# A gated two-network kernel: the hidden rows of the first network turned by VectorE and sixteen transfers a block instead of by TensorE

## The chip, the cores and the metric

One Trainium2 core runs the whole program in one launch. The metric is device microseconds (us) of an execution; the median of several runs stands for a kernel. Engines are named as in the profile: PE (TensorE matmul), PEld (its weight loads), DVE (VectorE), ACT (ScalarE), POOL (GpSimd) and SP (SyncE, which here only issues transfers).

## The reference

```python
for t in range(S):                                   # linear attention, 4 x 8 heads, S = 768, D = 48
    state = alpha[:, :, t, :, None] * state + einsum('bhd,bhe->bhde', k[:, :, t], v[:, :, t])
    y[:, :, t] = einsum('bhd,bhde->bhe', q[:, :, t], state)
...                                                  # x: 3072 tokens x 384
expert_idx = argmax(logits, axis=1)                  # one of 8 experts for each token
for e in range(8):                                   # first network
    h = maximum(x[mask] @ w1[e], 0.0)                # 384 -> 1024
    out[mask] = gate_w[mask, None] * (h @ w2[e])     # 1024 -> 384
h = out @ w_in                                       # second network, 384 -> 2048
return maximum(0.01 * h, h) @ w_out                  # 2048 -> 384
```

## The kernel before

The kernel has three stages: the attention (to about 120 us of the span), the first network (about 137 to 435 us) and the second network (to the end). The change lies in the first network.

Tokens are sorted by expert into 31 blocks (the code's windows) of 128 tokens. Every engine runs its own program over the 31 blocks, in a loop of two blocks a turn with a few blocks written out at either end, and semaphores order the engines. `w` is the block, `u` its parity, `half` one half (512) of the 1024 hidden features. For a block, in the order of the work:

- POOL gathers 128 rows of 384 (`gather`), PE turns them in three 128x128 pieces (`turn_gx`), ACT rounds them to the matmul's type (`gx_round`) and DVE takes the remainder (`gx_rest`), so that each product runs as three matmuls of parts.
- PE multiplies by w1 into two banks (`hidden`, 9 matmuls of 512 columns for each half), ACT writes the ReLU to `hs` (`relu`).
- PE turns `hs` in eight 128x128 pieces into two banks (`turn_h`), ACT rounds (line 780), DVE takes the remainder (line 1192); together these are `hT`.
- PE multiplies by w2 (`contract`, 24 matmuls of 384 columns), DVE copies the result (`ys`), POOL scatters it.

PE's step `w` runs `hidden(w+1)` half 0, `turn_h(w)`, `hidden(w+1)` half 1, `turn_gx(w+2)`, `contract(w)`. So one block is always ahead with w1.

Weights arrive as full floats in `raw` (two halves: w1 and w2 of an expert, 1.5 MB each) by SP's transfers, ACT rounds them in three pieces a half (`split_hi`) and DVE takes the remainders (`split_lo`) into one of two sets. SP issues the next half when DVE is through with the last one. The second network's weights come the same way as two more sets (`SET_IN`, `SET_OUT`), SP also loads the rows for the second network (`load_y`). The second network keeps PE on `inner` and `outward` in turn; its first two `inner` calls stand around the last `contract`.

Of the kernel before, what the change touches and what calls it, by code (L numbers as in the profile page):

```python
# [24 lines left out]
def build(nc, qka, v, emb, tau, w1, w2, w_in, w_out, x_dram, y_dram, gate_dram, out):  # L25
# [7 lines left out]
    E, _, F = w1.shape  # L33
    F2 = w_in.shape[1]
# [10 lines left out]
    assert F2 == 2 * F and SET_IN % 2 == 0 and E & (E - 1) == 0 and CH > 2 and BATCHES == 4 and L == P and WINDOWS % 2 == 1  # L45
# [22 lines left out]
    GW = gate_dram.shape[1]  # L68
    gate_rows = gate_dram.rearrange("(b c p) k -> b p c k", c=CH, p=P)
    o_rows = out.rearrange("(t p) d -> t p d", p=P)  # L70

    with ExitStack() as ctx:
# [25 lines left out]
        with ExitStack() as phase:  # L98
# [50 lines left out]
            wflag = sb("wflag", [P, 7, WINDOWS])  # L149
# [26 lines left out]
        with ExitStack() as phase:  # L176
# [13 lines left out]
            yf = sb("yf", [P, 2, GT])  # L190
            yT = sb("yT", [P, 2, 2, KD, GT], F32R)
            os_ = sb("os", [P, 2, TG, D])
# [49 lines left out]
        w_hi = sem("w_hi")  # L242
        w_lo = sem("w_lo")
# [30 lines left out]
        ht_turned = sem("ht_turned")  # L274
        ht_hi = sem("ht_hi")
# [72 lines left out]
        def each_window(eng, step, apart=0):  # L348

            for w in range(2 * apart):  # L350
                step(w, w % 2, True, True)
            with eng.Fori(apart, WINDOWS // 2 - 1) as i:
                for u in range(2):
                    step(i * 2 + u, u, True, True)
            for w in range(WINDOWS - 3, WINDOWS):
                step(w, w % 2, w + 1 < WINDOWS, w + 2 < WINDOWS)

        def table(eng, w):

            return eng.value_load(wtab[0:1, ds(w, 1)], min_val=0, max_val=8 * E - 1)  # L360
# [18 lines left out]
        def split_hi(act, n, par, pieces):  # L379
            for j in pieces:  # L380
                if j % 3 == 0:
                    act.wait_ge(raw_in[j // 3], n * 16 + 48)
                cols = slice(j * PC, (j + 1) * PC)
                act.activation(set_of(par, 0, cols), raw[:, cols], ACT.Copy).then_inc(w_hi, 1)  # L384

        def split_lo(dve, n, par, pieces):
            for j in pieces:
                dve.wait_ge(w_hi, n * PIECES + j + 1)
                cols = slice(j * PC, (j + 1) * PC)
                dve.tensor_tensor(set_of(par, 1, cols), raw[:, cols], set_of(par, 0, cols).bitcast(F32),  # L390
                                  ALU.subtract).then_inc(w_lo, 1)

        W1_PIECES, W2_PIECES = range(0, 3), range(3, 6)

# [3 lines left out]
        def _(sp):  # L398
# [24 lines left out]
            def load_half(half, src):  # L423
                h = slice(half * 3 * PC, (half + 1) * 3 * PC)
                sp.dma_start(raw[:, h].rearrange("p (k n) -> p k n", n=src.shape[2]), src).then_inc(raw_in[half], 16)

            def load_expert(e):
                sp.wait_ge(w_lo, (e - 1) * PIECES + 3)
                load_half(0, w1[ds(e, 1)].rearrange("a (k p) n -> p (a k) n", p=P))
                sp.wait_ge(w_lo, e * PIECES)  # L430
                load_half(1, w2[ds(e, 1)].rearrange("a (k p) n -> p (a k) n", p=P))

# [13 lines left out]
            def load_first(c):  # L446

                half, part = c // 3, c % 3
                if half == 0:
                    src, at = w1[0, part * P:(part + 1) * P], part * F  # L450
                    sp.dma_start(raw[:, at:at + F], src).then_inc(raw_in[half], 16)
                else:
                    ks = slice(part * HT // 3, (part + 1) * HT // 3)
                    dst = raw[:, 3 * PC + ks.start * D:3 * PC + ks.stop * D].rearrange("p (k n) -> p k n", n=D)
                    sp.dma_start(dst, w2[0, ks.start * P:ks.stop * P].rearrange("(k p) n -> p k n", p=P)).then_inc(raw_in[half], 16)
# [27 lines left out]
            with sp.Fori(1, E) as e:  # L483
                load_expert(e)
            for half in range(2):
                sp.wait_ge(w_lo, (SET_IN - 1) * PIECES + 3 * half + 3)
                load_half(half, w_in[:, half * F:(half + 1) * F].rearrange("(k p) n -> p k n", p=P))
# [17 lines left out]

            load_y(0, 0)
            load_y(1, 1)
            for half in range(2):
                sp.wait_ge(w_lo, SET_IN * PIECES + 3 * half + 3)
                load_half(half, w_out[half * F:(half + 1) * F].rearrange("(k p) n -> p k n", p=P))  # L510
# [13 lines left out]
        def _(pool):  # L524
# [86 lines left out]
            gather(0, slot_src[:, 2:3])  # L611
            pool.wait_ge(id_space, 1)

            def step(w, u, nxt, nxt2):
                nxt3 = not isinstance(w, int) or w + 3 < WINDOWS
                if nxt3:
                    pool.wait_ge(gx_turned, w + 2)
                    copy_index(w * 3 + 1, isrc, slot_src, w + 3, 1 - u)
                    gather(1 - u, isrc[:, 1 - u:2 - u])
# [3 lines left out]
                copies = w * 3 + 3 if nxt3 else WINDOWS - 3 + (w + 1) * 2  # L623
# [7 lines left out]
            each_window(pool, step)  # L631
# [24 lines left out]
        def _(act):  # L656
# [93 lines left out]
            def relu(w, u, half):  # L750
                act.wait_ge(h_ready, w * 2 + half + 1)
                act.activation(hs[:, u, half * HALF:(half + 1) * HALF], hps[u][half][:, :], ACT.Relu).then_inc(relu_done, 1)  # L752
# [10 lines left out]
            relu(0, 0, 1)  # L763
            act.wait_ge(tables_ready, 2)

            def y_round(t, u, k):
                act.wait_ge(yt_turned, t * KD + k + 1)
                act.activation(yT[:, u, 0, k], yf[:, (u * KD + k) % 2], ACT.Copy).then_inc(yt_hi, 1)

            def step(w, u, nxt, nxt2):  # L770
                code = table(act, w)
                e = act.snap((code & (E - 1)) + 1)
                early, late, second = (act.snap(code & (E << j)) for j in range(3))
                par = act.snap(e & 1)
                with act.If(early > 0):
                    wait_free(act, w)
                    split_hi(act, e, par, W1_PIECES)
                for half in range(2):
                    act.wait_ge(ht_turned, w * 2 + half + 1)
                    act.activation(hT[:, 0, half * HALF:(half + 1) * HALF], htps[half][:, :], ACT.Copy).then_inc(ht_hi, 1)  # L780
                if nxt:
                    relu(w + 1, 1 - u, 0)
                if nxt2:
                    gx_round(w + 2, u)
                if nxt:
                    relu(w + 1, 1 - u, 1)
                with act.If(late > 0):
                    wait_free(act, w)
                    split_hi(act, e, par, W1_PIECES)
                with act.If(second > 0):  # L790
                    split_hi(act, e, par, W2_PIECES)
# [3 lines left out]
                if nxt and not nxt2:  # L795
                    for k in range(KD):
                        y_round(0, 0, k)
                if not nxt:
                    split_hi(act, SET_OUT, 1, W1_PIECES)

            def wait_free(eng, w):

                eng.wait_ge(ye_ready, w + 1)

            each_window(act, step, 1)
# [45 lines left out]
        def _(dve):  # L851
# [136 lines left out]
            expert, differs, early, late, second, first, code = (wflag[:, j, :] for j in range(7))  # L988
# [610 lines left out]
```

## Time and profile before

| | us |
|---|---|
| median of 3 runs | 841.49 (841.44 to 842.94) |
| the profiled execution, its own time | 841.14 |
| its span in the trace | 839.4 |

| engine | busy us | share of the span |
|---|---|---|
| PE | 826.0 | 98% |
| PEld | 742.7 | 88% |
| DVE | 418.4 | 50% |
| ACT | 340.4 | 41% |
| POOL | 197.4 | 24% |

An execution takes 1.7 us more than its span. PE is busy nearly throughout, so what matters is which of its instructions are needed, and where another engine makes it wait.

### The profile page before, as it was taken

To read this page: it belongs to the slowest core of one execution; us is meant where nothing else is said; L and a number is where in the kernel's file an instruction comes from. 1 tells how busy PE (TensorE), PEld (TensorE's weight loads), DVE (VectorE), ACT (ScalarE), POOL (GpSimd) and SP (SyncE) were. 2 spreads that over 40 slices of the span, in tenths; PEclk is the share of its full clock that TensorE was granted. 3 is DMA by queue.
4 is the path that set the end of the run, shared out by engine and by line. 5 is a ranking of instruction groups with operands and counts; after the bars stand their busy time and mean duration, and the time that the engine had idled before them with its cause. 6 is when DMAs were issued, how large, how long until landed. Compare 5 with 4: busy or idle time off the path is not lost.

```text
span 839.4 us, 16998 instructions
## 1 busy us (share of the span) xinstructions
PE 826.0 (98%) x5491; PEld 742.7 (88%) x5492; DVE 418.4 (50%) x652; ACT 340.4 (41%) x643; POOL 197.4 (24%) x280
## 2 busy tenths in 40 slices
PE   7899999999999999999999999999999999999998
PEld 7788887999999999999999998998998998998997
DVE  7899986735544435445265433533533433443332
ACT  2545554634544425445254323323323333333223
POOL 6667623132233222332124003003003001000100
DMA  9988664435345332496002201201101000000001
GB/s 227 273 248 238 195 217 136 165 108 188 112 130 189 104 115 104 129 241 201 26 4 41 38 1 39 38 1 38 21 17 38 0 0 36 3 1 3 36 1 38
DMA packets 50454, 78.44 MB, mean 93 GB/s; under 512 B 22695, under 2 KB 39635, under 8 KB 50416
## 3 DMA queue, kind: packets, MB, share of 16 engines
q1 hardware_dynamic: 41232, 63.05, 26.1%
q0 software_dynamic: 5888, 14.85, 5.2%
q10 hardware_dynamic: 3296, 0.06, 0.2%
q8 instruction: 21, 0.34, 0.2%
q14 instruction: 17, 0.14, 0.1%
HBM read 63.69 MB, written 15.64 MB: 95 GB/s over the span
## 4 chain that ended last, share of the span: by engine, by line
PE 93%; DMA 3%; DVE 2%; POOL 1%; issue 1%; ACT 0%; SPq 0%; POOLq 0%; DVEq 0%
PE bank L1471 24%; PE bank L1506 24%; PE bank L1444 15%; PE bank L1424 15%; PE bank L1435 3%; DMA qkas<-qka 2%; PE bank L1266 2%; PE bank L1306 2%; PE bank L1283 2%; PE bank L1314 1%; PE bank L1400 1%; PE bank L1272 1%; PE bank L1326 1%; POOL kt L560 1%; DVE decay L874 0%
## 5 line engine op out<-in xcount | busy, mean ns | idle before, releaser
L1471 PE MATMUL bank<-yT,wts 128*128 128x512 f32 x864 | 217.0, 395 | 0.0
L1506 PE MATMUL bank<-wts,gs 128*128 128x384 f32 x1152 | 215.4, 335 | 0.4 <-ACT os L823 0.2
L1506 PEld LDWEIGHTS bank<-wts,gs 128*128 128x128 f32 x1152 | 202.1, 188 | 10.6 <-issue 1.6
L1471 PEld LDWEIGHTS bank<-yT,wts 128*128 128x128 f32 x864 | 160.7, 188 | 30.7
L1232 DVE TENSOR_TENSOR g<-bank,small 128x512 f32<-128x512 f32 x96 | 66.4, 692 | 174.1 <-ACT small L832 167.0
L1424 PE MATMUL bank<-wts,gxT 128*128 (+1 forms) x549 | 139.5, 398 | 0.2 <-issue 0.2
L1444 PE MATMUL bank<-wts,hT 128*128 x744 | 137.2, 339 | 0.0
L832 ACT ACTIVATE small<-bank 128x512 f32<-128x512 f32 x96 | 57.6, 600 | 187.3 <-PE bank L1471 165.7
L1444 PEld LDWEIGHTS bank<-wts,hT 128*128 128x128 f32 x744 | 128.5, 188 | 0.2
L1424 PEld LDWEIGHTS bank<-wts,gxT 128*128 128x128 f32 x549 | 100.2, 188 | 19.3 <-issue 0.8
L1234 DVE TENSOR_TENSOR gs<-g,gs 128x512 fp32r<-128x512 f32 x96 | 66.6, 693 | 67.0 <-ACT gs L835 61.5
L835 ACT ACTIVATE gs<-g 128x512 fp32r<-128x512 f32 x96 | 60.7, 632 | 72.9 <-DVE g L1232 68.3
L650 POOL DMA_INDIRECT out<-os,tokens x20 | 19.7, 987 | 288.0 <-ACT os L823 283.5
L780 ACT ACTIVATE hT<-bank 128x512 fp32r<-128x512 f32 x62 | 33.7, 597 | 122.6 <-PE bank L1435 122.6
L390 DVE TENSOR_TENSOR wts<-raw,wts 128x1024 f32 (+1 forms) x60 | 70.3, 1221 | 18.3 <-ACT wts L384 17.9
L627 POOL DMA_INDIRECT y_rows<-ys,idst x31 | 31.8, 1025 | 186.5 <-DVE ys L1218 186.5
L1192 DVE TENSOR_TENSOR hT<-bank,hT 128x512 fp32r<-128x512 f32 x62 | 39.9, 686 | 51.6 <-ACT hT L780 51.6
L384 ACT ACTIVATE wts<-raw 128x1024 f32 (+1 forms) x60 | 59.3, 1056 | 0.0
L752 ACT ACTIVATE hs<-bank 128x512 f32<-128x512 f32 x62 | 37.1, 599 | 4.5 <-PE bank L1424 2.4
L1218 DVE COPY ys<-bank 128x384 f32<-128x384 f32 x31 | 17.2, 554 | 41.0 <-PE bank L1444 40.9
L1057 DVE TENSOR_TENSOR gxT<-bank,gxT 128x384 fp32r<-128x384 f32 x30 | 16.7, 558 | 40.6 <-ACT gxT L748 40.6
L555 POOL TENSOR_TENSOR qt<-qkas,decay 112x512 f32<-112x512 f32 x24 | 30.7, 1281 | 19.3 <-DVE decay L874 17.9
(178 smaller groups left out, 728.9 us busy)
## 6 DMA issues: line engine op xcount, KB each, us to landing
raw<-w SPq DMA_DIRECT2D x14, 1536.0 KB, 7.2
qkas<-qka SPq DMA_DIRECT2D x20, 675.5 KB, 5.4
vs<-v SPq DMA_DIRECT2D x24, 192.0 KB, 3.8
x_rows<-xs SPq DMA_DIRECT2D x24, 192.0 KB, 3.9
yl<-y_rows SPq DMA_DIRECT2D x20, 192.0 KB
raw<-w_in SPq DMA_DIRECT2D x2, 1536.0 KB, 7.0
raw<-w_out SPq DMA_DIRECT2D x2, 1536.0 KB, 7.7
raw<-w SPq DMA_DIRECT2D x3, 512.0 KB, 5.5
```

The costliest lines, as they stand in the source:

```text
L384: act.activation(set_of(par, 0, cols), raw[:, cols], ACT.Copy).then_inc(w_hi, 1)
L390: dve.tensor_tensor(set_of(par, 1, cols), raw[:, cols], set_of(par, 0, cols).bitcast(F32), ALU.subtract).then_inc(w_lo, 1)
L752: act.activation(hs[:, u, half * HALF:(half + 1) * HALF], hps[u][half][:, :], ACT.Relu).then_inc(relu_done, 1)
L832: act.activation(small[:, f % 2], gps[f % 2][:, :], ACT.Copy, scale=0.01).then_inc(small_done, 1)
L835: act.activation(gs[:, f % 4, 0], g[:, f % 2], ACT.Copy).then_inc(g_hi, 1)
L1192: dve.tensor_tensor(hT[:, 1, h], htps[half][:, :], hT[:, 0, h].bitcast(F32), ALU.subtract).then_inc(ht_lo, 1)
L1232: dve.tensor_tensor(g[:, f % 2], gps[f % 2][:, :], small[:, f % 2], ALU.max).then_inc(g_done, 1)
L1234: dve.tensor_tensor(gs[:, f % 4, 1], g[:, f % 2], gs[:, f % 4, 0].bitcast(F32), ALU.subtract).then_inc(g_lo, 1)
L1424: m = pe.matmul(hps[u][half][:, :], gxT[:, u, x_part, k * P:(k + 1) * P], set_of(par, w_part, slice(n, n + HALF)), start=(k == 0 and (x_pa ...
L1444: m = pe.matmul(yeps, hT[:, h_part, k * P:(k + 1) * P], set_of(par, w_part, slice(n, n + D)), start=(k == 0 and (h_part, w_part) == (0, 0) ...
L1471: m = pe.matmul(gps[f % 2][:, :], wts[:, 0, w_part, n:n + P], yT[:, u, y_part, k], start=(k == 0 and (w_part, y_part) == (0, 0)), stop=(k ...
L1506: m = pe.matmul(ops[tt], gs[:, f % 4, g_part, tt * P:(tt + 1) * P], wts[:, 1, w_part, f * D:(f + 1) * D], start=(f == 0 and (g_part, w_par ...
```

## The change

From block 2 on (`FIRST = 2`) PE no longer turns the hidden rows. ACT writes the ReLU of a half to a buffer `hr`; DVE turns that half in squares of 32x32 within each group of 32 partitions (`turn_h`, now on DVE) into `hs`; SP brings the squares to their partitions with sixteen transfers of 32 partitions x 256 floats (32 KB) from `hs` to `hds` (`move_h`); ACT rounds and DVE takes the remainder out of `hds` instead of out of the banks. PE runs `hidden` two blocks ahead: step `w` is `hidden(w+2)` both halves, `turn_gx(w+3)`, `contract(w)`. Blocks 0 and 1 are still turned by PE. `hds` and `hr` lie where the second network's `yT` has its slot 0, so that network starts with slot 1. Weights are laid out on the host as one array with 12 KB in a row for each partition and half; ACT issues their transfers, right behind its rounding of the half before, and waits there for DVE's third remainder (`load_half`). Only the two halves of expert 1 are still issued by SP. w1 and w2 have semaphores of their own, and the table of flags that says when to split which half is made in fewer steps. Both `inner` calls now stand ahead of the last `contract`.

```diff
-            with sp.Fori(1, E) as e:
-                load_expert(e)
             for half in range(2):
+                load_half(sp, half, 1)
+            def move_h(w, u):
+                for j in range(QUADS):
+                    if j % 2 == 0:
+                        sp.wait_ge(h_turned, (w - FIRST) * 2 + j // 2 + 1)
+                    if j == 0 and not (isinstance(w, int) and w < FIRST + 2):
+                        sp.wait_ge(ht_lo, w * 2 - 2)
+                    for i in range(QUADS):
+                        sp.dma_start(hds[j * SQ:(j + 1) * SQ, u, i * QF:(i + 1) * QF],
+                                     hs[i * SQ:(i + 1) * SQ, u, j * QF:(j + 1) * QF]).then_inc(h_moved[u], 16)
...
+            move_pairs(FIRST // 2 + 1, 10)
             load_y(0, 0)
+            move_pairs(10, 13)
             load_y(1, 1)
...
+                act.activation(hr[:, half], hps[u][half][:, :], ACT.Relu).then_inc(relu_done, 1)
+            def h_round(w, u, half):
...
+                act.wait_ge(h_moved[u], w * 128 - 128 * u)
+                act.wait_ge(ye_ready, w + 1)
+                act.activation(by_square(hT[:, 0, cols]), moved(u, half), ACT.Copy).then_inc(ht_hi, 1)
+            def first_weights(s, e):
+                wait_from(act, h_ready, s * 2)
+                split_hi(act, e, next_set(act, e), W1_PIECES)
+                load_half(act, 0, next_expert(act, e))
...
             relu(0, 0, 1)
+            first_weights(0, 1)
             act.wait_ge(tables_ready, 2)
...
+            def turn_h(w, u):
                 for half in range(2):
+                    dve.wait_ge(relu_done, w * 2 + half + 1)
+                    dve.transpose(hs[:, u, half * HALF:(half + 1) * HALF].rearrange("p (n f) -> p n f", f=SQ),
+                                  hr[:, half].rearrange("p (n f) -> p n f", f=SQ)).then_inc(h_turned, 1)
...
+            def step(w, u):
+                if isinstance(w, int) and w == 0:
+                    block_hidden(1, 1)
+                if isinstance(w, int) and w < FIRST:
+                    turn_h(w, u)
+                if isinstance(w, int) and w == 0:
+                    turn_gx(2, 0)
+                if ahead(w, 2):
+                    block_hidden(w + 2, u)
+                if ahead(w, 3):
+                    turn_gx(w + 3, 1 - u)
+                if not ahead(w, 1):
...
+                    for f in range(2):
+                        inner(0, 0, f)
...
                 contract(w, u, par)
```

On PE, in a block of the loop before, the end of the first half's matmuls, the turning of the hidden rows (`bank45<-ident,hs`) and the start of the second half's stand so:

```order
L1424 MATMUL bank23<-wts,gxT 128x512 x2
L1432 ISA
L1435 MATMUL bank45<-ident,hs 128x128 [waits relu_done]
L1435 MATMUL bank45<-ident,hs 128x128 x3
L1432 REGISTER_ALU
L1435 MATMUL bank45<-ident,hs 128x128 [waits relu_done]
L1435 MATMUL bank45<-ident,hs 128x128 x3
L1424 ISA
L1424 MATMUL bank23<-wts,gxT 128x512
```

On PE after the change, at block 0's step, written out: the turning of block 0's hidden rows is followed by the turning of block 2's gathered rows (`ident,xg`) and then by a wait for those rows' remainder.

```order
L1510 MATMUL bank45<-ident,hs 128x128 [waits relu_done]
L1510 MATMUL bank45<-ident,hs 128x128 x7
L1475 MATMUL bank7<-ident,xg 128x128 [waits gx_lo,gathered0]
L1475 MATMUL bank7<-ident,xg 128x128 x2
L377 TENSOR_LOAD wtab
L377 ISA x2
L1555 REGISTER_ALU [waits gx_lo]
L1555 ISA
L1499 REGISTER_ALU [waits relu_done,w1_lo]
```

So the eight turning matmuls are gone from the loop, and in block 0's step the w1 matmuls of block 2 now stand ahead of block 0's `contract`.

On ACT after the change, ahead of the loop: the rounding of expert 1's w1 (`wts<-raw`, with its wait for the transfer) and the issue of the next transfer (with its wait for DVE) stand ahead of the ReLU of block 1 (`hs<-bank23`).

```order
L799 ACTIVATE hs<-bank1 128x2x8x32 [waits h_ready]
L401 ACTIVATE wts<-raw 128x1024 [waits raw_in0]
L401 ACTIVATE wts<-raw 128x1024 x2
L415 DMA raw<-weights 128x3072 [waits w1_lo]
L799 ACTIVATE hs<-bank23 128x2x8x32 [waits h_ready,tables_ready]
L799 ACTIVATE hs<-bank23 128x2x8x32 [waits h_ready]
```

Before, that rounding stood in block 0's step behind the rounding of `hT` and the ReLU of block 1, and no transfer was issued by ACT there.

On SP after the change, a block of the loop is sixteen transfers, with a wait ahead of each eight:

```order
L520 ISA [waits h_turned]
L522 DMA hds_52<-hs 32x256 [waits ht_lo]
L522 DMA hds_52<-hs 32x256 x7
L518 REGISTER_ALU
L522 DMA hds_52<-hs 32x256 [waits h_turned]
L522 DMA hds_52<-hs 32x256 x7
```

Before, SP's loop held two transfers of 1.5 MB an expert and nothing else.

## Rows read from the trace of the kernel before

**Rows 1.** The page's part 1: span, then busy us, share, instructions of PE.
```profile
span 839.4 us, 16998 instructions
...
PE 826.0 (98%) x5491; PEld 742.7 (88%) x5492; DVE 418.4 (50%) x652; ACT 340.4 (41%) x643; POOL 197.4 (24%) x280
```
**Rows 2.** The chain that ended last, in order of time: start us, us, what.
```profile
166.56 4.19 PE bank L1444 x24
170.74 2.08 PE bank L1424 x9
173.70 2.08 PE bank L1424 x9
176.11 4.19 PE bank L1444 x24
```
**Rows 3.** Groups by line: busy us, mean ns of one, idle before.
```profile
L1435 PE MATMUL bank<-ident,hs 128*128 128x128 f32 x248 | 32.1, 272 | 0.0
...
L1108 DVE STREAM_TRANSPOSE yf<-yl 128x512 f32<-128x512 f32 x18 | 12.6, 704 | 0.0
```
**Rows 4.** SP's queue in order of time: start us, us, transfers issued.
```profile
363.93 10.13 SPq L503 DMA_DIRECT2D yl<-y_rows  x8
...
603.38 7.45 SPq L500 DMA_DIRECT2D yl<-y_rows  x16
```
**Rows 5.** SP's line 417: ns of an issue, least/median/most, first and last start.
```profile
L417 SPq DMA_DIRECT2D vs<-v x24: 332/384/649, 3.6 to 104.9; - x24
```
**Rows 6.** Timeline at the first blocks: start us, us, engine, line.
```profile
137.67 27.48 SPq L425 DMA_DIRECT2D raw<-w  x4
...
141.76 2.31 PE L1424 MATMUL bank<-wts,gxT 128*128 x9 [0.24 <-issue]
...
144.54 1.09 ACT L780 ACTIVATE hT<-bank 128x512 fp32r<-128x512 f32 x2 [2.38 <-PE bank L1435]
...
147.37 0.49 ACT L748 ACTIVATE gxT<-bank 128x384 fp32r<-128x384 f32 x1 [1.25 <-PE bank L1400]
...
147.90 0.56 DVE L1057 TENSOR_TENSOR gxT<-bank,gxT 128x384 fp32r<-128x384 f32 x1 [1.44 <-ACT gxT L748]
148.24 2.95 ACT L384 ACTIVATE wts<-raw 128x1024 f32 x3
...
151.53 3.50 DVE L390 TENSOR_TENSOR wts<-raw,wts 128x1024 f32 x3 [0.41 <-ACT wts L384]
```
**Rows 7.** Transfers issued from 137 to 139 us: KB each, us to landing.
```profile
raw<-w SPq DMA_DIRECT2D x1, 1536.0 KB, 6.9
```
**Rows 8.** PE's timeline in the first stage and at 122 us.
```profile
2.97 5.06 PE L1257 MATMUL bank<-ones 128*128 128x128 f32 x22 [2.97 <-POOL prio L544]
...
9.20 1.16 PE L1266 MATMUL bank<-qt,kt 48*128 48x128 f32 x16
...
12.30 1.16 PE L1266 MATMUL bank<-qt,kt 48*128 48x128 f32 x16 [1.40 <-POOL kt L560]
...
122.51 4.20 PE L1257 MATMUL bank<-ones 128*128 128x128 f32 x36
```
**Rows 9.** Timeline where the second network begins.
```profile
435.35 4.36 PE L1471 MATMUL bank<-yT,wts 128*128 128x512 f32 x18
435.62 0.56 DVE L1218 COPY ys<-bank 128x384 f32<-128x384 f32 x1 [1.19 <-PE bank L1444]
435.76 0.60 ACT L832 ACTIVATE small<-bank 128x512 f32<-128x512 f32 x1 [3.00 <-DVEq L1223]
436.39 0.69 DVE L1232 TENSOR_TENSOR g<-bank,small 128x512 f32<-128x512 f32 x1 [0.22 <-ACT small L832]
```
**Rows 10.** The stretch of the first network: busy us, granted clock, DMA share, GB/s.
```profile
137.00:430.00 293.00, 292.76 (x1620) 265.11 (x1620) 141.94 (x222) 128.00 (x209) 75.50 (x147) 1.00 0.43 138
```
**Rows 11.** ACT's timeline: the first of two weight splits of two experts in a row.
```profile
186.56 2.95 ACT L384 ACTIVATE wts<-raw 128x1024 f32 x3
...
215.22 2.95 ACT L384 ACTIVATE wts<-raw 128x1024 f32 x3
```

More of the change, by code:

```diff
@@ L32, in build @@
     N, D = v.shape
-    E, _, F = w1.shape
-    F2 = w_in.shape[1]
+    E, F = weights.shape[0] - 2, 1024
+    F2 = 2 * F
     BATCHES = 4
@@ L448, in load_first @@
                 half, part = c // 3, c % 3
[L449 to L455, printed above, removed]
+                sp.dma_start(raw[:, c * PC:(c + 1) * PC],
+                             weights[0, half, :, part * PC:(part + 1) * PC]).then_inc(raw_in[half], 16)
             def step(c, b):
@@ L767, in y_round, with step @@
                 act.wait_ge(yt_turned, t * KD + k + 1)
[L768 to L777, printed above, removed]
-                for half in range(2):
[L779 to L791, printed above, removed]
+                act.activation(yT[:, 1 - u, 0, k], yf[:, (u * KD + k) % 2], ACT.Copy).then_inc(yt_hi, 1)
+            def step(w, u):
+                if isinstance(w, int) and w == 0:
+                    for half in range(2):
+                        relu(1, 1, half)
+                    e, first = follower(act, 1)
+                    with act.If(first > 0):
+                        first_weights(1, e)
+                for half in range(2):
+                    h_round(w, u, half)
+                if isinstance(w, int) and w == 0:
+                    gx_round(2, 0)
+                if ahead(w, 2):
+                    for half in range(2):
+                        relu(w + 2, u, half)
+                if ahead(w, 3):
+                    gx_round(w + 3, 1 - u)
+                if ahead(w, 2):
+                    e, first = follower(act, w + 2)
+                    with act.If(first > 0):
+                        first_weights(w + 2, e)
+                e, first = follower(act, w)
+                with act.If(first > 0):
+                    second_weights(w, e)
                 if isinstance(w, int) and w == 1:
@@ L987, in _ @@
             W = WINDOWS
-            expert, differs, early, late, second, first, code = (wflag[:, j, :] for j in range(7))
+            expert, first, code = (wflag[:, j, :] for j in range(3))
             start("side", dve.memset(cx, 0.0))
-            start("side", dve.memset(differs, 1.0))
             start("side", dve.memset(first, 1.0))
@@ L1201, in step @@
                     make_gates()
-                with dve.If(late > 0):
-                    split_lo(dve, e, par, W1_PIECES)
-                with dve.If(second > 0):
-                    split_lo(dve, e, par, W2_PIECES)
-                if nxt and not nxt2:
+                if ahead(w, 2):
+                    e, first = follower(dve, w + 2)
+                    with dve.If(first > 0):
+                        split_lo(dve, e, next_set(dve, e), W1_PIECES)
+                e, first = follower(dve, w)
+                with dve.If(first > 0):
+                    split_lo(dve, e, next_set(dve, e), W2_PIECES)
+                if isinstance(w, int) and w == WINDOWS - 2:
                     y_turn(0, 0, 0)
```

238 lines of the change are left out of this document (134 added, 104 removed).

## Prediction, made before the changed kernel ran

> **What bounds the kernel now.** I read the page's busy shares first: PE is busy 826.0 of 839.4 us [rows 1]. A share says little about a stage, so next the stretch of the first network: 292.76 of 293 us, at a granted clock of 1.00, while DVE has 142 and ACT 128 us of work [rows 10]. Nothing there makes PE wait; whatever leaves PE's program shortens the stage, as long as no one else becomes late. Third, the chain that ended last, in order of time, gives a block's anatomy [rows 2]: `contract` 4.19, `hidden` half 0 2.08, then a hole of 0.88 (170.74 + 2.08 = 172.82, and the next group starts at 173.70), half 1 2.08, then 0.33 up to 176.11. The holes are the turnings that the list merges away: eight of `hs`, three of the gathered rows. A block's period is 176.11 - 166.56 = 9.55 us.
>
> The group of line 1435 says 32.1 us for 248 turnings [rows 3]. That counts overlapping instructions twice (0.272 x 8 = 2.2 us a block, where the chain leaves 0.88), so the chain's figure is the one to use.
>
> **What goes.** The turnings of blocks 2 to 30, 29 blocks at 0.88: 25.5 us off PE. A block then takes 4.19 + 4.16 + 0.33 = 8.67 us.
>
> **What that asks of the others, a block.**
> - DVE: two more transposes at 0.70 [rows 3], the same size as the second network's. With the two remainders of `hT` (0.69 for this size [rows 9]), the gathered remainder (0.56 [rows 6]) and `ys` (0.56 [rows 9]) that is 3.9 us; with one half of weights, 3.50 more [rows 6], 7.4.
> - ACT: two ReLUs and two roundings at 0.60 or less, one gathered rounding at 0.49: 2.9 us. A weight half adds 2.95, the wait for DVE's third piece (about one piece, 3.50 / 3 = 1.2) and an issue of about 0.4 [rows 5]: 7.4. An expert has three or four blocks here (the first splits of two experts are 28.7 us, three periods, apart [rows 11]); w1 is split two blocks ahead of the step that splits w2, so the two never share a step.
> - SP: sixteen issues. No row has a transfer of 32 runs of 1 KB. Sixteen of 128 runs each took 7.45 us, 0.466 each; eight of 512 runs 10.13, 1.27 each [rows 4]. Longer lists cost more, so the first is the nearest from above, and 0.33, the cheapest issue [rows 5], is the lower end. I take 0.466: 7.45 us of the 8.67.
>
> All three fit, SP with only 1.2 us to spare. Does a moved block come in time? Counted from the start of step w-2: half 0 out of PE at 2.08, ReLU 0.60, transpose 0.70, so SP starts at 3.4 and has issued all at 10.9. For the landing I bound from 0 to 6.9, that of a 1.5 MB weight transfer [rows 7]: at most 17.8. It is needed when ACT must begin rounding for `contract(w)`, which starts at 2 x 8.67 + 4.5 = 21.8; less 0.60 and 0.69 that is 20.5. So the moves are hidden, with 2.7 us left at the worst landing. In a step with a weight half ACT and DVE end about 1.5 us late; PE has 4.5 us of `hidden` to cover 1.3 of rounding and remainder, so that is hidden too.
>
> **What is put on the path at the start.** ACT's order is where I expect the loss. Ahead of block 1's ReLU it now waits for expert 1's w1, issued at 137.67 [rows 6] and landing 6.9 later [rows 7], at 144.6. From there: three roundings with DVE one piece behind, 1.0 + 3.5, to 149.1; the issue, 149.5; two ReLUs of block 1, 150.7; two roundings of block 0's `hT`, 1.09, 151.8; the rounding of block 2's gathered rows, 0.49, and DVE's remainder, 0.56 [rows 6], 152.9; with handoffs of about 0.1 each, 153.5. PE meanwhile starts block 1's `hidden` at 141.76 [rows 6] and runs out after 4.16 + 0.88 + 0.33, at 147.1: it needs block 2's remainder. **Loss 6.4 us.** In block 1's step a second one: ACT has to wait for DVE, which does block 0's small table work and w2's remainders first; ACT comes free some 0.6 us after PE wants block 1's `hT`. **0.6.** If w1 landed at once, the first would shrink to about 3; if it landed 2 us later, grow to 8.4.
>
> **The clock.** PE's first eleven products of ones, sent as 22 instructions, took 5.06 us, 0.230 each, behind 2.97 us in which it had nothing to do; the same form at 122.51, in a busy stretch, takes 4.20 / 36 = 0.117 [rows 8]. So that opening ran at the lower of the two levels, 1.2 GHz, and the rest at 2.4, though the printed clock is 1.00 throughout. After an idle time of 1.40 us the score products took the same 1.16 us as before it [rows 8]. 6.4 us of idling lies nearer to the opening: I charge its 5.06 us at half rate, **2.5 us**; the other end is 0. The Trainium skill, "TensorE: Matmul & The Clock Gate", Part 1, says the slow state is the default and activity releases it; by that rule the 2.5 belong in the sum, and the opening agrees.
>
> **At the end.** Block 29 has no `hidden` beside it any more (block 30's came in step 28) and `hT` has one buffer: after `contract(28)` PE waits for ACT's half, 0.60, and DVE's, 0.69, with handoffs **1.5**. And since both `inner` calls now precede the last `contract`, the third one, which needs DVE's first `g`, has no cover: before, 435.35 to 437.08 was hidden under PE's 4.36 us [rows 9]; now PE waits from the end of `contract` (435.5) to the end of `g` (437.08), **1.6**.
>
> **At nothing:** the flag table (some eight small DVE instructions fewer, beside PE's first `hidden`), the layout of the weights (their landing is waited for at the start alone, counted above at the old 6.9), and the slot of `yT`.
>
> **Sum**, against the profiled execution's 841.1 (the median is 0.35 above it): 841.1 - 25.5 + 6.4 + 0.6 + 2.5 + 1.5 + 1.6 = **828.2 us**. A difference under 0.2%, 1.7 us, can't be told from none.
>
> **Rivals.**
> 1. *The clock stays up over the stall at the start.* For it: no row shows a fall in mid-program. Against: the opening. 828.2 - 2.5 = 825.7. Chance 0.22.
> 2. *Moved blocks come late behind the second network's loads.* SP issues four y transfers between blocks 19 and 20, and again between 25 and 26: 10.13 / 2 = 5.1 us [rows 4]. The next block's moves are then issued at 16.0; with a landing of 6.9, 22.9 against 20.5, so PE waits 2.4, and SP regains 1.2 a block. Twice: 833.0, some more if a weight transfer falls in as well. For it: the DMA share, 0.43 before [rows 10], gains 0.5 MB a block. Against: small transfers should land sooner than 1.5 MB. Chance 0.15.
> 3. *Slower: SP becomes the bound.* Place: its queue, in all 29 blocks. With 16 issues of p and some 0.3 of waits a block, the net gain of 12.9 is gone when 16p + 0.3 = 8.67 + 12.9 / 29, p = 0.552. At 0.649, the slowest issue in a busy queue [rows 5], a block takes 10.7 and the kernel 828.2 + 29 x 2.0 = 887. For it: an issue waits when its queue can't take more, as the 1.27 shows; and the moves share the engines with weights on another queue. Against: 32 runs are few. Chance 0.10. The Trainium skill, "DMA: Bandwidth & Descriptors", "Rules for kernel authors", speaks against the change here: transfers under 64 KB pay mostly overhead and should be merged; these are 32 KB. By that rule the cost lies per transfer, as in this rival; the sixteen of 7.45 us neither confirm nor exclude it, being 48 KB.
>
> That PE doesn't lose the turnings at all is excluded: they are gone from its loop. The forecast has 0.48; 0.05 is for what I don't see. The range, 822 to 838, holds the forecast, rivals 1 and 2, a stall at the start 3 us longer or shorter, and two y loads that cost twice as much; it leaves out rival 3. The floor, with no new wait at all, is 841.1 - 25.5 = 815.6. Faster: 0.48 + 0.22 + 0.15 = 0.85; slower: rival 3 and some of the rest, 0.12; same: 0.03.
>
> **What would show it.** In the chain, a block of 8.67 with no hole between two groups of nine; a larger one refutes the main term, and SP's queue without gaps between its sixteens would name rival 3. A wait of PE near 147 us, released by DVE's gathered remainder, of 6.4; the nine-matmul groups behind it near 4 us instead of 2.08 for the clock. Waits of 1.5 and 1.6 about the last two blocks. `hT` roundings on ACT released by a transfer, rather than by PE, would be rival 2. The prediction fails most likely on SP's issue time, which no row shows for this shape.

## The result: SP became the bound

The changed kernel takes 896.6 us (median of 4 runs, 895.4 to 899.7) where the kernel before takes 841.5: ratio 1.0657, 95% interval 1.0625 to 1.0689. The forecast was 828.2, faster. What happened is its third rival in its outcome, SP as the bound; it had a chance of 0.10 and a price of 887.

The page of the changed kernel: span, the engines' shares, the granted clock in 40 slices of the span, then part 4 (the chain that ended last, by engine).

```profile
span 895.8 us, 17320 instructions
...
PE 819.2 (91%) x5259; PEld 732.4 (82%) x5260; DVE 450.6 (50%) x702; ACT 341.4 (38%) x643; POOL 206.0 (23%) x279
...
PEclk9999998999899899899898999999999999999999
...
PE 57%; SPq 27%; issue 4%; DVE 4%; DMA 4%; ACT 1%; POOL 1%; ACTq 0%; DVEq 0%; POOLq 0%
```

Against [rows 1] PE has less work and is idle more: the 826.0 busy us fell to 819.2 only, mainly because some `contract` groups now run on a lower clock (the row of PEclk has eights in the first network's slices, where the clock was 1.00 before [rows 10]), and PE waits 52.7 us for `hT`. The chain says for whom: 27% of the span is SP issuing, in a chain where its share was 0% before. DVE is busy for 450.6 us (418.4 before) and ACT for 341.4 (340.4), so neither of them is the bound.

SP's queue in order of time (start, us, transfers issued), which answers [rows 4]:

```profile
159.12 197.53 SPq L522 DMA_DIRECT2D hds<-hs  x288
356.92 4.68 SPq L544 DMA_DIRECT2D yl<-y_rows  x4
361.91 64.65 SPq L522 DMA_DIRECT2D hds<-hs  x96
426.83 4.51 SPq L544 DMA_DIRECT2D yl<-y_rows  x4
431.66 52.65 SPq L522 DMA_DIRECT2D hds<-hs  x80
```

One line's issues (ns, least/median/most), which answers [rows 5]:

```profile
L522 SPq DMA_DIRECT2D hds<-hs x464: 507/591/1570, 159.1 to 483.7; - x155
```

From 159 us on SP does hardly anything but issue. Its last two rows of moves give 52.65 / 80 = 0.658 and 64.65 / 96 = 0.673 us from one issue to the next, of which 0.591 (the median) is the instruction. From the first issue to the last the 29 blocks take (483.7 - 159.1) / 29 = 11.2 us each: sixteen issues at 0.66 to 0.67 make 10.5 to 10.8, the y loads between them (4.68 + 4.51 us) 0.3 a block, the rest is SP's waits. PE's program would need 8.65.

A stretch of the changed kernel's timeline (start, us, engine, line; in brackets the idle time before and what ended it):

```profile
295.47 16.57 SPq L522 DMA_DIRECT2D hds<-hs  x25
298.80 1.15 ACT L814 ACTIVATE hT<-hds 128x512 fp32r<-128x512 f32 x2 [9.81 <-DMA hds<-hs]
299.46 1.29 DVE L1252 TENSOR_TENSOR hT<-hds,hT 128x512 fp32r<-128x512 f32 x2 [8.02 <-ACT hT L814]
...
300.51 6.10 PE L1519 MATMUL bank<-wts,hT 128*128 x24 [6.27 <-DVE hT L1252]
...
306.45 4.29 PE L1499 MATMUL bank<-wts,gxT 128*128 x18
```

The chain in one picture: SP issues without a gap, ACT stands 9.81 us until the last squares are in, DVE behind ACT, PE 6.27 us behind DVE. The `contract` that follows takes 6.10 us; where PE doesn't wait it takes 4.44 (shown below for e9_four). The idling costs a second time, through the clock: the granted clock is 0.69 over this `contract`, a mixture of its two levels of 1.2 and 2.4 GHz, and 1.00 over the 18 matmuls behind it. Not every wait does this: behind 2.43 and 2.34 us the same 24 matmuls took 4.42 and 4.44, behind 1.98 us 6.00, and behind each of the five waits of 6.05 us or more 6.10 to 6.90.

PE's waits in the changed kernel (us in total, times, longest):

```profile
PE bank L1519 <- DVE hT L1252: 52.7, 19, 10.1
PE bank L1499 <- DVE gxT L1126: 6.2, 1, 6.2
...
PE bank L1519 <- DVE hT L1249: 2.4, 1, 2.4
PE bank L1546 <- DVE g L1307: 1.6, 1, 1.6
```

The other three lines are the forecast's terms at the start (6.4 expected), in block 1 (0.6 expected) and ahead of the third `inner` (1.6 expected).

### The profile page after: what moved, and what is told of

Read it like the earlier page. It is cut to its first block, busy times and chain, and to the rows that moved or that the text cites. A ratio compares the mean times of both kernels' runs of the same rounds, so it can differ in the third digit from the quotient of the medians.

```text
span 895.8 us, 17320 instructions
## 1 busy us (share of the span) xinstructions
PE 819.2 (91%) x5259; PEld 732.4 (82%) x5260; DVE 450.6 (50%) x702; ACT 341.4 (38%) x643; POOL 206.0 (23%) x279
## 4 chain that ended last, share of the span: by engine, by line
PE 57%; SPq 27%; issue 4%; DVE 4%; DMA 4%; ACT 1%; POOL 1%; ACTq 0%; DVEq 0%; POOLq 0%
SPq L522 26%; PE bank L1546 23%; PE bank L1590 22%; PE bank L1341 2%; PE bank L1381 2%; PE bank L1358 2%; PE bank L1519 2%; DMA qkas<-qka 2%; PE bank L1499 1%; PE bank L1389 1%; SPq L544 1%; DMA hds<-hs 1%; PE bank L1347 1%; DVE wts L407 1%; DMA raw<-weights 1%
## 5 line engine op out<-in xcount | busy, mean ns | idle before, releaser
L1519 PE MATMUL bank<-wts,hT 128*128 x744 | 149.0, 359 | 55.3 <-DVE hT L1252 52.7
L1519 PEld LDWEIGHTS bank<-wts,hT 128*128 128x128 f32 x744 | 139.5, 203 | 60.9 <-issue 60.9
L1499 PE MATMUL bank<-wts,gxT 128*128 (+1 forms) x549 | 132.7, 396 | 6.2 <-DVE gxT L1126 6.2
L1499 PEld LDWEIGHTS bank<-wts,gxT 128*128 128x128 f32 x549 | 103.7, 190 | 27.2 <-issue 6.4
L814 ACT ACTIVATE hT<-hds 128x512 fp32r<-128x512 f32 x58 | 33.4, 623 | 177.2 <-DMA hds<-hs 153.7
L1252 DVE TENSOR_TENSOR hT<-hds,hT 128x512 fp32r<-128x512 f32 x58 | 37.6, 689 | 91.1 <-ACT hT L814 87.4
L401 ACT ACTIVATE wts<-raw 128x1024 f32 (+1 forms) x60 | 59.4, 1053 | 9.9 <-issue 8.1
L1242 DVE STREAM_TRANSPOSE hs<-hr 128x512 f32<-128x512 f32 x58 | 38.3, 690 | 14.4 <-ACT hr L804 14.4
L804 ACT ACTIVATE hr<-bank 128x512 f32<-128x512 f32 x58 | 31.9, 586 | 17.4 <-PE bank L1499 17.4
```

The lines of the kernel that those rows point to most:

```text
L1242: dve.transpose(hs[:, u, half * HALF:(half + 1) * HALF].rearrange("p (n f) -> p n f", f=SQ), hr[:, half].rearrange("p (n f) -> p n f", f=S ...
L1499: m = pe.matmul(hps[u][half][:, :], gxT[:, u, x_part, k * P:(k + 1) * P], set_of(par, w_part, slice(n, n + HALF)), start=(k == 0 and (x_pa ...
L1519: m = pe.matmul(yeps, hT[:, h_part, k * P:(k + 1) * P], set_of(par, w_part, slice(n, n + D)), start=(k == 0 and (h_part, w_part) == (0, 0) ...
```

## The experiments

**The theory after the result:** an issue from SBUF to SBUF costs SP about 0.6 us, whatever it carries; sixteen a block are more than a block. Rivals: the queue is full and the issue waits for its drain (then the bytes or the number of runs, the contiguous pieces that a transfer lists, decide); or the squares simply land late. In the ratios below the kernel before, run beside each, has a median of 840.2 to 841.1 us; a ratio can lie up to 0.4% off the quotient of the two medians.

### e1_act4: a quarter of the issues on ACT

```diff
-                for j in range(QUADS):              # SP's move_h
+                for j in range(QUADS - 1):
...
+                    act_moves(w + 2, u)             # ACT: the four transfers of j = 3, behind gx_round(w + 3)
```

> The last four of a block's sixteen transfers are issued by ACT instead of SP; their number, bytes and data stay. Issue theory (SP spends about 0.65 us on each, 16 x 0.65 = 10.5 us a block): SP needs 12 x 0.65 = 7.9, so PE's 8.67 bounds the block again apart from steps in which ACT also splits weights; 835 us, between 828 and 850. Drain theory (the transfer engines can't take the moved squares faster, and SP's issue is only held up by that): the same transfers take the same time whoever issues them, 897 us. Theory that the other parts of the change cost the time: also about 897.

Measured: 916.4 us, ratio 1.0904 (1.0858 to 1.0950): slower still, and the expectation of 835 missed by far. ACT's issues (ns, least/median/most), then a step with weights from its timeline:

```profile
L822 ACTq DMA_DIRECT2D hds<-hs x116: 514/613/838, 160.9 to 491.2; - x116
```

```profile
304.67 2.69 ACTq L822 DMA_DIRECT2D hds<-hs  x4
...
308.45 2.96 ACT L401 ACTIVATE wts<-raw 128x1024 f32 x3 [4.25 <-issue]
309.77 3.50 DVE L407 TENSOR_TENSOR wts<-raw,wts 128x1024 f32 x3 [4.77 <-ACT wts L401]
...
314.81 1.15 ACT L814 ACTIVATE hT<-hds 128x512 fp32r<-128x512 f32 x2 [3.40 <-issue]
...
316.52 6.50 PE L1529 MATMUL bank<-wts,hT 128*128 x24 [4.36 <-DVE hT L1262]
```

An issue on ACT is no cheaper (0.613 median), and it stands in ACT's program: four of them, 2.69 us, push back the rounding of the weights, DVE behind it, and the rounding of `h` behind that. SP's twelve fit now, at 0.591 each as before; in their place ACT became the bound in 15 steps (58.5 us of PE's waits). What I had not costed is whose work stands behind the moved issues. The cost of an issue itself is confirmed, the remedy refuted.

### e2_wide and e3_dram_src: the same bytes in fewer issues, the same issues from memory

In short form:

```diff
-  hds[j*SQ:(j+1)*SQ, u, i*QF:(i+1)*QF] <- hs[i*SQ:(i+1)*SQ, u, j*QF:(j+1)*QF]           # 16 x 32 KB
+  hds[64 partitions, u, i*QF:(i+1)*QF] <- hs[64 partitions, u, n*QF:(n+1)*QF]            # e2_wide: 8 x 64 KB
+  hds[j*SQ:(j+1)*SQ, u, i*QF:(i+1)*QF] <- x_dram[32 rows, 0:QF]                          # e3_dram_src: 16 x 32 KB
```

> Eight transfers of 64 partitions x 256 floats a block instead of sixteen of 32, the same 512 KB; squares then land on wrong partitions, so the hidden rows are not those of the reference. Issue theory: if an issue still takes about 0.65, SP needs 5.2 us a block, PE is the bound, 830 us (826 to 836); if an issue of 64 runs takes twice as long, 897. Drain theory: same bytes, same runs, 890 to 897.

> The sixteen transfers keep number, shape and destination but read the gathered tokens' array in memory instead of the turned rows, so the hidden rows are not those of the reference. It measures the issue by itself: if the 0.59 us come from both sides lying in SBUF, an issue falls to the 0.43 of the old loads from memory and the kernel to about 830; if they come from the instruction's shape (32 rows of 1 KB) or its place in the loop, it stays at 0.59 and the kernel at 897.

Measured: e2_wide 844.1 us (ratio 1.0039, 1.0023 to 1.0055), e3_dram_src 845.7 in one run (its reading here is the price of an issue, not the time). The issues, first of e2_wide, then of e3_dram_src (ns, least/median/most):

```profile
L522 SPq DMA_DIRECT2D hds<-hs x232: 461/597/1619, 159.4 to 422.8; - x116
```

```profile
L522 SPq DMA_DIRECT2D hds<-x_rows x464: 310/422/1355, 159.5 to 428.1; - x155
```

Twice the bytes and twice the runs in one transfer cost SP the same, 0.597; the same shape read from memory costs 0.422. So it is neither the drain nor the list's length, but a price for each instruction, and a higher one where both sides lie in SBUF. The two transfers a block of e5_trip (below), each of 512 KB with one side in memory, bear this out: their medians are 0.326 for the store from SBUF and 0.370 for the load into SBUF, a load of 512 runs. At 0.422 sixteen fit into a block, and of the 52.7 us of waits 10.7 are left (11.5 in e2_wide). Yet both kernels stay 16 to 17 us above the forecast, at the time of before: with SP out of the way the rest of the change is worth nothing.

### e4_pe_turns: everything but the moves

PE turns `hs` of all blocks as before (`turn_h`), nothing is moved, the rest of the change stays.

> PE turns the hidden rows of all blocks, no squares and no transfers; all the rest of the change stays (two blocks ahead, weights issued by ACT, one semaphore for each half, both inner calls first). Issue theory and drain theory both: a block takes the old 9.55 us, plus the start's 6.2 and about 2 for the slow clock behind it, 0.6, and 1.5 and 1.6 at the end: 853 us (849 to 856). Theory that the other parts cost the time: near 897.

Measured: 856.3 us, ratio 1.0190 (1.0158 to 1.0222). By the forecast's terms it should be 841.1 + 6.4 + 0.6 + 2.5 + 1.5 + 1.6 = 853.7. So what the change puts on the path apart from the moves is 15 us, 2.6 more than costed. The steps with weights are not in this figure: with the turnings back PE waits for `hT` in blocks 1 and 29 alone (2.2 and 1.3 us).

### e5_trip and e6_sp_loads: squares by way of memory, weights on SP

```diff
+                sp.dma_start(h_dram[u], hs[:, u]).then_inc(h_stored, 16)
+                sp.wait_ge(h_stored, w * 16 - 16)
+                sp.dma_start(hds[:, u]..., h_dram[u].rearrange("(i c) (j q) -> (c j) i q", ...)).then_inc(h_moved[u], 16)
...
-                load_half(act, 0, next_expert(act, e))      # e6_sp_loads: issued by SP behind the block's load
+                    load_half(sp, half, next_expert(sp, e))
```

> The 16 transfers of a block are replaced by two: one store of the turned block (512 KB) to a scratch tensor in memory, and one load that brings the squares to their partitions (features then lie on the partitions in another order, and w2's rows are laid out to match; the output stays the reference's). Issue theory (SP needs 0.59 us for each issue between two places in SBUF, 0.65 with the gap behind it, whatever lies in it): two issues a block are some 1.2 us of 8.65, PE's waits for hT shrink to what e2_wide and e3_dram_src showed (some 11 us in 13 steps), kernel 839 to 846 us. Rival (it is the bytes in DMA engines and SBUF that are slow, and these double here to 1 MB a block): PE still waits in most blocks, kernel 870 us or more. A third way: store and load one behind the other land too late for the block two steps on; then every block waits some us, kernel 850 to 870.

> As e5_trip, and the next expert's weights are loaded from SP's queue (behind the block's store and load) instead of ACT's. Theory: the 11 us of small waits (13 steps, up to 1.8 us) that were left in e2_wide and e3_dram_src come from ACT, which waits with its issue for DVE's third piece of the weights (ACT's last piece ends at 297.2 in e2_wide, DVE's at 299.1, the issue 299.3 to 299.7, and only then the rounding of h begins). With the issue on SP they go: kernel 829 to 834 us, PE's waits for L1252's counterpart under 2 us. Rival: the pieces themselves (2.96 us on ACT, 3.5 on DVE in one step) are too much for these steps, and DVE is late whoever issues: the waits stay at 8 to 11 us, kernel 839 to 845.

Measured: e5_trip 849.6 us (ratio 1.0120, 1.0080 to 1.0159), a little over its range; e6_sp_loads 858.0 (1.0237, 1.0170 to 1.0305), where 829 to 834 was expected. SP's queue in e6_sp_loads, then the issues of SP and ACT about a block of e5_trip:

```profile
406.57 0.35 SPq L416 DMA_DIRECT2D raw<-weights  x1
407.08 0.34 SPq L518 DMA_DIRECT2D h_rows<-hs  x1
416.08 0.37 SPq L522 DMA_DIRECT2D hds<-h_rows  x1
419.40 0.32 SPq L518 DMA_DIRECT2D h_rows<-hs  x1
423.00 0.38 SPq L522 DMA_DIRECT2D hds<-h_rows  x1
```

```profile
265.26 0.36 ACTq L416 DMA_DIRECT2D raw<-weights  x1
269.02 0.33 SPq L518 DMA_DIRECT2D h_rows<-hs  x1
275.81 0.37 SPq L522 DMA_DIRECT2D hds<-h_rows  x1
```

With two issues a block the queue is nearly empty of work, but the store issued 0.5 us behind 1.5 MB of weights is through only 9.0 us later (416.08 - 407.08), where the next one, long behind the weights, takes 3.6; PE waits for that block. SP was relieved and the block's latency took its place. The rival named for e6_sp_loads is not what happened either: ACT's rounding of `h` waits there 59.4 us in 12 steps for the loaded squares, not for DVE's pieces. That the common queue is the reason is not shown. In e5_trip the weights go out on ACT's queue, and the store 3.8 us behind them takes 6.8 us; counted from the issue of the weights, both stores are through after about the same time, 9.5 us on one queue and 10.5 on two. What e6_sp_loads changed for certain is that the weights stand closer ahead of the store.

### e7_start and e8_end: first tries on that base

e7_start adds another order at the start, e8_end one at the end of the first network (both are used again below, the second in a changed form).

> As e6_sp_loads, with another order at the start: PE turns block 2's gathered rows ahead of block 1's first stage, ACT and DVE round them there, the pieces of expert 1's w1 come behind block 0's roundings (ahead of them only where block 1 is already expert 1's), and DVE places the slots before block 0's rest. Theory: PE's stall of 6.2 to 6.4 us ahead of block 2's first stage goes, with it the slow clock behind it (1.95 us) and most of block 1's 2.4 us: 9 to 11 us less than e6_sp_loads, about 821 us. Rival: something else is late there (the gather of block 2, whose rows land some 3 us behind its issue at 138, or the weights' pieces now late for block 4): half of it or less, 825 us or more.

> As e7_start, and at the end of the first network the first group's y rows are turned and rounded one step earlier, the second network's first inner product stands ahead of block 29's contraction (where PE waited 1.8 us for hT) and its second behind block 30's (behind which PE waited 1.6 us for g). Theory: of these 3.4 us some 1.4 stay (block 30's hT has nothing to hide it), so 2 us less than e7_start, about 819 us. Rival: the turned y rows now delay DVE's rest of block 29 by as much: no difference.

Measured: 859.1 us (ratio 1.0179, 1.0125 to 1.0234) and 856.7 (1.0208, 1.0164 to 1.0252): neither can be told from e6_sp_loads by its interval. So neither gave what was expected of it. In e7_start the stall for block 2's remainder went, as it should; PE waits in its place 2.8 us for block 2's gathered rows, which come beside 3 MB of weights (held back in e11_start below, where this wait is gone), and as in e6_sp_loads for `hT` (16.9 us in 7 steps; 16.6 in 7 there), where the late squares decide.

### e9_four: four transfers a block

```diff
-                for j in range(QUADS):
...
-                    for i in range(QUADS):
-                        sp.dma_start(hds[j * SQ:(j + 1) * SQ, u, i * QF:(i + 1) * QF],
-                                     hs[i * SQ:(i + 1) * SQ, u, j * QF:(j + 1) * QF]).then_inc(h_moved[u], 16)
...
+                for i in range(QUADS):
+                    sp.dma_start(hds[:, u, i * QF:(i + 1) * QF], hs[i * SQ:(i + 1) * SQ, u]).then_inc(h_moved[u], 16)
```

A transfer's elements are taken in order on either side: 32 partitions of 1024 become 128 of 256. Partition 4c + j then holds feature c of quarter j, and w2's rows are laid out on the host to match.

> The changed kernel with 4 transfers a block in place of 16, still between two places in SBUF: each takes 32 partitions of the turned block with 4 KB a partition and lays them on all 128 partitions with 1 KB each (features then lie on the partitions in another order, and w2's rows are laid out to match, so the output stays the reference's). Issue theory: 4 issues of 0.6 us are 2.4 of 8.65 us; SP is no bound, and what stays is what e2_wide showed (some 11 us of small waits in the steps with weights, 6.4 us at the start, 2.4 in block 1, 1.6 at the end): 840 to 846 us, less than e5_trip's 849.6, since the bytes go once and not twice. Rival (an issue's time grows with what it writes, so that 4 issues of 128 runs take what 16 of 32 took): SP is the bound again, 890 us.

Measured: 841.8 us, ratio 1.0026 (1.0012 to 1.0039). Its issues, then PE's waits:

```profile
L520 SPq DMA_DIRECT2D hds<-hs x116: 542/605/1685, 160.4 to 420.4; - x116
```

```profile
PE bank L1516 <- DVE hT L1249: 10.5, 13, 1.8
PE bank L1496 <- DVE gxT L1123: 6.5, 1, 6.5
...
PE bank L1516 <- DVE hT L1246: 2.4, 1, 2.4
PE bank L1543 <- DVE g L1304: 1.6, 1, 1.6
```

128 KB an issue, 0.605 us: the price is for the instruction. With the same bytes and twelve issues fewer a block the kernel goes from 896.6 to 841.8. The Trainium skill, "Perfetto Trace Analysis", "What 'DMA-bound' means", lists this bound, an issuing engine whose track is solid with transfers, and recommends large descriptors; the trace agrees with the diagnosis, and the cure here was fewer instructions (e2_wide kept the runs of 1 KB and halved the instructions).

What is left is the steps with weights. PE's `contract` groups in e9_four, then what ACT, DVE and SP do in one such step:

```profile
254.34 4.44 PE L1516 MATMUL bank<-wts,hT 128*128 x24
263.89 4.44 PE L1516 MATMUL bank<-wts,hT 128*128 x24 [0.66 <-DVE hT L1249]
272.54 4.44 PE L1516 MATMUL bank<-wts,hT 128*128 x24
281.96 4.43 PE L1516 MATMUL bank<-wts,hT 128*128 x24 [0.53 <-DVE hT L1249]
```

```profile
256.54 2.96 ACT L401 ACTIVATE wts<-raw 128x1024 f32 x3 [1.26 <-issue]
257.95 3.50 DVE L407 TENSOR_TENSOR wts<-raw,wts 128x1024 f32 x3 [1.86 <-ACT wts L401]
...
261.61 0.36 ACTq L415 DMA_DIRECT2D raw<-weights  x1
262.14 1.15 ACT L811 ACTIVATE hT<-hds 128x512 fp32r<-128x512 f32 x2 [2.64 <-DVE wts L407]
...
262.81 1.33 DVE L1249 TENSOR_TENSOR hT<-hds,hT 128x512 fp32r<-128x512 f32 x2 [0.90 <-ACT hT L811]
```

Without weights a block takes 272.54 - 263.89 = 8.65 us (8.67 predicted); with them, in this step, 263.89 - 254.34 = 9.55. ACT's three pieces end at 259.50, but it stands 2.64 us (issue included) until DVE is through and the next load is issued, and only then rounds `h`. The 1.26 us ahead of the pieces, which the profile calls `issue`, are ACT's own program: it reads the table of flags twice and branches on it,

```profile
L377 ACTq TENSOR_LOAD <-wtab x2: 273/278/282, 254.7 to 255.5; - x2
```

and the forecast charged nothing for that. A wait of 0.66 costs 0.90: each new stall costs about 0.24 more than its label, since where PE doesn't wait a `contract` starts 0.24 us before the recorded end of the turning ahead of it.

### e10_defer, e11_start, e12_end: taking the rest away

```diff
                 split_hi(act, e, next_set(act, e), W1_PIECES)
-                load_half(act, 0, next_expert(act, e))
...
+                    load_next(w + 1, 0)                     # e10_defer: in the next step, behind h_round
+                    load_next(w - 1, 1)                     # and between the two halves of ReLU
...
+                    turn_gx(2, 0)                           # e11_start: PE, ahead of block_hidden(1, 1)
                     block_hidden(1, 1)
-            first_weights(0, 1)                             # ACT: now behind h_round(0), unless block 1 needs it
+            gx_round(2, 0)
+            for rows, blocks in zip(gathered, (2, 1)):      # SP: block 2's rows ahead of expert 1's weights
...
-                    for f in range(2):                      # e12_end: inner 0 ahead of contract(29), inner 1 behind contract(30),
-                        inner(0, 0, f)                      # h's first half rounded at the middle of the contract before
```

> As e9_four, and ACT issues the load of the next weights one step later than it rounds these (behind the roundings of h, between the two halves of ReLU), from its own queue as before, so that it doesn't stand waiting for DVE's third piece and the squares don't queue behind 1.5 MB on SP's queue, as they did in e6_sp_loads (where hT waited for the loaded squares 59.4 us in 12 steps). Theory: the small waits for hT (10.7 to 11.5 us in 13 steps) fall under 4 us: 8 us less than e9_four, 832 to 836 us. Rival: DVE's own 3.5 us in these steps, not ACT's stall, makes hT late: 2 us less at most, 838 or more.

> As e10_defer, with the order at the start of e7_start, and SP's loads of expert 1's weights held until block 2's rows are gathered (in e7_start and e8_end PE waited 2.75 us for these rows, which landed at 145.5 beside 3 MB of weights). Theory: the stall of 6.4 us ahead of block 2's first stage, the 1.9 us of slow clock behind it and most of block 1's 2.4 us go, and nothing comes in their place: 9 to 11 us less than e10_defer, 822 to 826 us. Rival: the rows are late without the weights too, or expert 1's weights now land too late for block 4: 828 us or more.

> As e11_start, with the end of the first network in another order (the first group's y rows turned and rounded in block 27's step, the second network's first inner product ahead of block 29's contraction, its second behind block 30's), and the first half of h rounded as soon as the contraction before has read its own first half (a semaphore on the matmul in its middle). Theory: in e11_start PE waits 1.8 us for block 29's hT, runs its contraction at the slow clock behind that (6.01 for 4.35 us), waits 1.6 us for the first g and some 2.5 us in small gaps: 3 to 5 us less than e11_start in the same run's terms, ratio to before 0.975 to 0.979, some 820 to 822 us. Rival: block 30's hT, with nothing ahead of its contraction now, costs what the others gave (1.5 us, and a slow clock of 1.6 behind it): ratio 0.980 to 0.983, no less than e11_start's 0.9816 by more than 0.1%.

Measured: e10_defer 835.2 us (ratio 0.9939, 0.9923 to 0.9956), e11_start 825.2 (0.9816, 0.9789 to 0.9842), e12_end 823.0 (0.9785, 0.9762 to 0.9809). The first two fell into their ranges; the third's ratio does too (not its 820 to 822 us), but its interval reaches into e11_start's, so its 0.3% is not shown. The same kind of step in e10_defer:

```profile
254.54 2.96 ACT L401 ACTIVATE wts<-raw 128x1024 f32 x3 [1.26 <-issue]
...
257.40 1.14 ACT L811 ACTIVATE hT<-hds 128x512 fp32r<-128x512 f32 x2
...
259.94 0.36 ACTq L415 DMA_DIRECT2D raw<-weights  x1
...
260.99 4.40 PE L1527 MATMUL bank<-wts,hT 128*128 x24
```

ACT rounds `h` right behind its last piece (257.40) and issues the load 2.5 us later; PE waits for nothing there. In seven other places 3.3 us of waiting are left that the profile puts down to no other engine (the `issue` line below). PE's largest waits in e10_defer:

```profile
PE bank L1507 <- DVE gxT L1134: 6.6, 1, 6.6
...
PE bank L1527 <- issue: 3.3, 7, 0.7
...
PE bank L1527 <- DVE hT L1260: 1.8, 1, 1.8
...
PE bank L1527 <- DVE hT L1257: 1.6, 1, 1.6
```

In e12_end 4.1 us of `issue` in ten places and 1.6 us for one `hT` are left in `contract`, and the wait for the first `g` is gone.

## Why the prediction was wrong, point by point

Two rows for the points below: a line's issues in the kernel before (point 1; ns, least/median/most) and PE's restart in the changed kernel (point 4).

```profile
L503 SPq DMA_DIRECT2D yl<-y_rows x20: 303/490/2897, 363.9 to 537.4; - x20
```

```profile
153.69 6.11 PE L1499 MATMUL bank<-wts,gxT 128*128 x18 [6.19 <-DVE gxT L1126]
```

1. **The step that failed: SP's price for an issue, "Sixteen of 128 runs each took 7.45 us, 0.466 each ... I take 0.466".** Those sixteen come out of memory; the moves go from SBUF to SBUF. Measured 0.591 for the instruction and 0.66 to 0.67 with the gap behind it, over the break-even of 0.552 that rival 3 gave. e2_wide and e9_four show that the length of the list, which I took for the reason of a higher or lower price, makes none here (0.597 and 0.605 for two and four times the bytes); e3_dram_src shows that where the ends lie does (0.422 for the same shape out of memory). The row behind "longer lists cost more" was misread too: 1.27 is a mean over a stretch with a few long issues, not the price of one. The median of that line is 0.490. The sentence at the end, that it fails most likely there, named the right place; the chance of 0.10 was too small for a term with 1.2 us to spare and a price taken from another kind of transfer.
2. **Rival 3: right in its outcome, not in its reason.** 887 by a price of 0.649; measured 896.6. The sixteens cost what it says (10.5 to 10.8 a block); the rest of the 11.2 is y loads and waits. That the price fits is luck: 0.649 was one slow issue of another line [rows 5], and the reason given, an issue that waits when its queue can't take more, is not what the runs show. In e9_four, where SP has nothing to issue for most of a block, an issue takes 0.605 all the same.
3. **What goes from PE: right.** 8.65 us a block without weights (8.67), seen in e9_four.
4. **The start: right.** A wait of 6.2 us (6.4), with ACT's first piece at 144.63 (144.6) and PE's restart at 153.69 (153.5). The slow clock: in the changed kernel the 18 matmuls behind the stall take 6.11 us where later ones take 4.29, so 1.8 (2.5 charged); rival 1, no loss, is out. e11_start took these away, with what was left of block 1's wait: 10.0 us less than e10_defer.
5. **Block 1: 2.4 us for 0.6**, and **the steps with weights: "that is hidden too"** is wrong. In e9_four PE waits 10.5 us for `hT` in 13 steps; 1.8 of it is block 29's (point 6), the other 8.7 fall in 12 steps with weights. I had summed ACT's work (7.4 us of a block, the wait for DVE included) and not asked where in ACT's program the rounding of `h` stands: behind that wait. e10_defer, which moves only that issue, gives 6.6 us back, and takes block 1's wait from 2.4 to 1.6; what made the rest of block 1's wait was not taken apart.
6. **The end: right.** 1.8 us ahead of `contract(29)` (1.5) and 1.6 for the third `inner` (1.6).
7. **Rival 2** can't be read from the changed kernel, whose queue is never empty. In e9_four, with four issues a block, no rounding of `h` waits for a transfer, and PE waits for nothing in the blocks next to the y loads (loads at 322.97 and 377.84, `contract` at 326.87 and 381.70). Four y loads take SP 2.0 us there, not the 5.1 charged.

The account closes on e9_four against before, by the trace: 29 x (9.55 of before - 8.65) = 26.1 us gained; lost 6.5 at the start, about 1.5 of clock (5.75 us for the 18 matmuls), 2.4, 1.6, 10.5, and 0.24 for each of 16 new waits, 3.8: 26.3 in all. The spans differ by 0.2 us (839.6 and 839.4). What the account leaves out is small: the first network starts 0.4 us earlier in e9_four (135.63 against 136.05).

## What to carry to other kernels

Price an issue by where both of its ends lie, and count issues, not bytes: four transfers that take 32 partitions to 128 did what sixteen did, once the features' order was free to change. When a sum leaves an in-order engine 86% full, look at what stands behind each of its waits, and ask the same of the engine to which you move work: moved to ACT a quarter of the issues made the kernel slower, and one issue put behind the urgent rounding instead of ahead of it gave 6.6 us. A gain off the bound engine can be spent wholly at the edges (here 26 us of 26), so the start, the end and the odd steps are to be costed like the loop.

## What the runs showed of the hardware

- An issue from SBUF to SBUF took SP 0.591, 0.597 and 0.605 us (medians) at 32, 64 and 128 KB, and ACT 0.613 at 32 KB. With one end in memory it was less: 0.422 for a load of 32 KB in the same shape (e3_dram_src), 0.326 for a store and 0.370 for a load of 512 KB (e5_trip).
- A transfer whose two sides have other numbers of partitions (32 x 1024 to 128 x 256) takes one issue like any other (0.605, e9_four).
- A store of 512 KB issued 0.5 us behind 1.5 MB on the same queue took 9.0 us, one 3.8 us behind 1.5 MB on the other queue 6.8, one long behind them 3.6.
- Reading an entry of the table of flags took ACT 0.273 to 0.282 us. Ahead of the roundings of weights ACT stands up to 1.3 us for such readings and the branches behind them (11.6 us in 11 places in e9_four), which the profile shows as `issue`.
